# First expert tile from the first eleven token tiles, records loaded one tile deeper, another stage order in the head

## The reference

```python
# token phase, both parts
scores = scale * np.matmul(q_c, k_c.transpose(0, 1, 2, 4, 3))      # chunks of 64 of 576, 8 x 8 heads, d = 64
attn = softmax(scores)                                              # written out in the reference, eps 1e-9
x = (attn @ v_c), laid out as 4608 tokens x 512
r = np.maximum(x @ w_in, 0.0)                                       # 512 -> 2048
x2 = (s * (r * r) + b) @ w_out                                      # 2048 -> 512
# expert phase
do_compute = x2 @ w_skip > 0
logits = x2[do_compute] @ w_gate                                    # 8 experts
e_idx, gate_w = argmax(logits), softmax(logits) at e_idx
for e in range(8):
    y = gate_w * (np.maximum(x2[of e] @ w1[e], 0.0) @ w2[e])        # 512 -> 1024 -> 512
    out[of e] = x2[of e] + y
out[not do_compute] = x2
```

## Time and profile before

| | us |
|---|---|
| median of 3 runs | 1430.13 |
| lowest, highest | 1428.49, 1430.82 |
| the profiled execution | 1431.54 |
| its span in the trace | 1429.8 |

### The profile page before, as it was taken

One profiled execution on the slowest core, in us unless ns is written; L12 is line 12 of the kernel. 1 busy time (PEld: TensorE's weight loads), 2 busy tenths in 40 slices (PEclk: granted clock), 3 DMA queues, 4 the chain that ended last, 5 costly groups with the idle time before them and its releaser, 6 DMA issues.

```text
span 1429.8 us, 22258 instructions
## 1 busy us (share of the span) xinstructions
PE 1338.8 (94%) x7002; PEld 1175.2 (82%) x7003; DVE 937.3 (66%) x2130; ACT 776.3 (54%) x1900; POOL 339.4 (24%) x284
## 2 busy tenths in 40 slices
PE   3699999999999999999999999998578899999998
PEld 3698999989898989889898989997466777888887
DVE  3586878878796878778786978756355655233332
ACT  5696766657575757666575756543344543222221
POOL 4552222122222222121222222101121222111111
PEclk9899999999999999999999999999799999999999
DMA  5142212112031203112121302023454641111110
GB/s 210 67 148 89 100 34 91 44 40 93 31 100 27 94 23 100 35 62 69 42 93 29 104 19 89 31 95 126 154 184 153 239 162 37 44 39 42 43 44 25
DMA packets 61459, 116.25 MB, mean 81 GB/s; under 512 B 11704, under 2 KB 20920, under 8 KB 61216
## 3 DMA queue, kind: packets, MB, share of 16 engines
q1 hardware_dynamic: 40816, 73.51, 15.8%
q10 hardware_dynamic: 14416, 27.79, 5.6%
q0 software_dynamic: 6112, 13.56, 2.9%
HBM read 90.49 MB, written 27.08 MB: 82 GB/s over the span
## 4 chain that ended last, share of the span: by engine, by line
PE 72%; issue 10%; DMA 6%; POOL 5%; DVE 4%; ACT 2%; DVEq 1%; POOLq 0%; ACTq 0%; SPq 0%
PE h_ps L645 22%; PE y_ps L660 22%; PE y_ps L763 10%; PE h_ps L750 8%; PE s_ps L608 3%; DMA wide<-x_rows,got 3%; PE av_ps L626 3%; POOL qk_lo L491 2%; DMA got<-table 2%; POOL table L510 2%; PE t_ps L743 1%; PE t_ps L616 1%; ACT soft L834 1%; PE av_ps L757 1%; DVE weights_lo L1024 1%
## 5 line engine op out<-in xcount | busy, mean ns | idle before, releaser
L1051 DVE CUSTOM_DVE_ANT_0 products<-scratch,wide 128x512 f32<-128x512 f32 x297 | 302.3, 1018 | 6.6
L645 PE MATMUL h_ps<-rows_t_hi,weights_lo 128*128 128x384 f32 x768 | 261.5, 340 | 7.3 <-issue 5.5
L864 ACT ACTIVATE scratch<-h_ps 128x384 f32<-128x384 f32 x192 | 94.5, 492 | 307.2 <-PE h_ps L645 305.2
L645 PE MATMUL h_ps<-rows_t_hi,weights_hi 128*128 128x384 f32 x768 | 260.6, 339 | 0.0
L645 PE MATMUL h_ps<-rows_t_lo,weights_hi 128*128 128x384 f32 x768 | 259.2, 337 | 0.0
L660 PE MATMUL y_ps<-weights_hi,g_lo 128*128 128x512 f32 x576 | 227.1, 394 | 0.6 <-DVE g_lo L1030 0.6
L660 PE MATMUL y_ps<-weights_hi,g_hi 128*128 128x512 f32 x576 | 226.7, 394 | 0.0
L660 PE MATMUL y_ps<-weights_lo,g_hi 128*128 128x512 f32 x576 | 226.5, 393 | 0.0
L1030 DVE TENSOR_TENSOR g_lo<-scratch,g_hi 128x384 fp32r<-128x384 f32 x192 | 109.3, 570 | 104.0 <-ACT g_hi L812 101.7
L491 POOL TENSOR_TENSOR qk_lo<-qk_raw,qk_hi 128x768 fp32r<-128x768 f32 x66 | 128.4, 1945 | 146.0 <-ACT qk_hi L812 146.0
L645 PEld LDWEIGHTS h_ps<-rows_t_hi,weights_lo 128*128 128x128 f32 x768 | 145.2, 189 | 21.1 <-issue 7.1
(11 more groups left out here) (168 smaller groups left out, 2445.4 us busy)
## 6 DMA issues: line engine op xcount, KB each, us to landing
qk_raw<-in_qk SPq DMA_DIRECT2D x66, 384.0 KB, 3.0
expert_raw<-in_w ACTq DMA_DIRECT2D x32, 512.0 KB, 5.0
scratch<-in_w ACTq DMA_DIRECT2D x21, 512.0 KB, 5.3
out<-scratch SPq DMA_DIRECT2D x12, 768.0 KB, 4.2
x_rows<-scratch SPq DMA_DIRECT2D x12, 768.0 KB, 6.0
v_raw<-in_v SPq DMA_DIRECT2D x66, 128.0 KB, 2.1
expert_raw<-in_w SPq DMA_DIRECT2D x11, 512.0 KB, 3.8
wide<-in_w_out SPq DMA_DIRECT2D x7, 512.0 KB, 4.1
```

The lines of the kernel that those rows point to most:

```text
L645: mm = pe.matmul(h_ps[f % 2][:, 0:TOK], w[:, f // PAIR, kt, fs], x[:, z, kt, :], start=kt == 0 and n == 0, stop=kt == KT - 1 and n == 2)
L864: act.activation(r_buf[f % 2], h_ps[f % 2][:, 0:TOK], ACT.Relu).then_inc(r_done, 1)
L1051: dve.tensor_tensor_reduce(products[:, :], x2_sb[:, t, :], gate_w[:, e, :], 1.0, 0.0, ALU.mult, ALU.add, logits[:, t, e:e + 1]).then_inc(d ...
```

## The change

1. **Head.** The orders of the stages per step are B, D, C instead of D, B, C on the matmul engine, A, D, C, B instead of D, A, C, B on ScalarE, and B, D, C, B2 instead of D, B, C, B2 on VectorE.
2. **Token tiles.** ScalarE takes stage A ahead of the parts of g in slot 1. The last value product stands after 3 instead of 6 matmuls of its slot's `into_h`. In the last token tile routing of tile 10 is finished in slot 9 instead of 14, with three dots a slot.
3. **First expert tile.** Expert tile 0 takes the first 128 records of expert 0 as they stand after eleven token tiles. `next_row` of expert 0 is raised to at least 128, so that later tokens go to the next expert tile; expert 0 gets at least two tiles. Its records are loaded and its rows gathered within the last token tile, and it is computed between the logits and the bounds of that tile, written out as straight code. The loops over experts begin at expert tile 1.
4. **Records.** A new copy `idx` of the records serves the gather, so that `got` is free as soon as `idx` is taken, and SP loads records one tile ahead. VectorE makes the copy (`next_records`), at the end of `stage_rows`, after a wait on its own two copies and on the record load.
5. **Weights.** Expert 1's first three pieces are loaded at the start of the last token tile, the fourth ahead of the last store, pieces 4 to 6 after it; the staging places of expert 0 move accordingly. The order of the last loads on SP is new; ScalarE's queue no longer issues four of them between the phases.

The diff, cut to its core:

```diff
@@ tensor
-                for stage, c in first_chunks(step, ("D", "B", "C")):
+                for stage, c in first_chunks(step, ("B", "D", "C")):
@@ scalar
-                for stage, c in first_chunks(step, ("D", "A", "C", "B")):
+                for stage, c in first_chunks(step, ("A", "D", "C", "B")):
-                    order = "DCgAB" if f == FT - 1 else "CgADB"
+                    order = {1: "AgCDB", FT - 1: "DgCAB"}.get(f, "CgADB")
@@ vector
-                for stage, c in first_chunks(step, ("D", "B", "C", "B2")):
+                for stage, c in first_chunks(step, ("B", "D", "C", "B2")):
@@ tensor, slot 14
-                        into_h(i, f + 1, z, range(KT // 2))
+                        into_h(i, f + 1, z, range(1))
                         attention("D", CPT * (i + 1) + CPT - 1, CPT - 1)
-                        into_h(i, f + 1, z, range(KT // 2, KT))
+                        into_h(i, f + 1, z, range(1, KT))
@@ routing's slots
-        RANK_AT = 14
+        RANK_AT = {True: 14, False: 9}
...
+                by.append(min(by[-1] + (3 if f % 2 or not attend else 1), DOTS))
@@ sync
             sp.wait_ge(av_done, CPT * TILES)
-            for j in range(EXPERT_JOBS):
-                if j >= 2:
-                    sp.wait_ge(raw2_done, j - 1)
-                load_weights(sp, 0, j)
-            store_rows(TILES - 1)
-            sp.wait_ge(raw2_done, EXPERT_JOBS)
+            sp.wait_ge(x_ready, CPT * TILES)
+            load_weights(sp, 0, 0)
+            load_weights(sp, 0, 1)
             for j in range(3):
                 load_weights(sp, 1, j)
-
-            def load_records(tile, row):
-
-                sp.wait_ge(got_free, tile + 1)
-                sp.dma_start(got[:, :], table[bass.ds(row, P), :]).then_inc(got_in, 16)
-
+            for j in range(2, EXPERT_JOBS - 1):
+                sp.wait_ge(raw2_done, j - 1)
+                load_weights(sp, 0, j)
+            sp.wait_ge(records_out, 16 * SUB * (TILES - 1))
+            load_records(0, 0)
+            sp.wait_ge(raw2_done, EXPERT_JOBS - 2)
+            load_weights(sp, 0, EXPERT_JOBS - 1)
+            sp.wait_ge(raw2_done, EXPERT_JOBS - 1)
+            load_weights(sp, 1, 3)
+            store_rows(TILES - 1)
+            sp.wait_ge(x2_stored, 32 * TILES)
+            sp.wait_ge(tail_done, 1)
+            for j in range(4, EXPERT_JOBS - 1):
+                load_weights(sp, 1, j)
+            sp.wait_ge(bounds_ready, 1)
+            first_end = sp.value_load(bounds[0:1, 1:2], min_val=2, max_val=N // P + E)
             sp.wait_ge(records_out, 16 * SUB * TILES)
-            sp.wait_ge(bounds_ready, 1)
-            with sp.Fori(0, E) as e:
+            with sp.Fori(1, first_end) as t:
+                load_records(t, t * P)
+            with sp.Fori(1, E) as e:
...
@@ gpsimd
-            send_records(TILES - 2)
-            send_records(TILES - 1)
-            pool.memset(x_rows, 0.0).then_inc(rows_held, 16)
+            def gather(count, stored):
+                pool.wait_ge(x2_stored, 32 * stored)
                 pool.wait_ge(rows_held, count)
                 pool.indirect_dma_start(
-                    in_offset=bass.IndirectOffsetOnAxis(ap=got[:, 0:1].bitcast(U32), axis=0),
+                    in_offset=bass.IndirectOffsetOnAxis(ap=idx[:, 0:1].bitcast(U32), axis=0),
...
-            pool.wait_ge(bounds_ready, 1)
-            gather(16)
-            pool.dma_start(y_rows, x2_rows[0:P, :]).then_inc(y_free, 16)
-            gather(32)
+            send_records(TILES - 2)
+            pool.wait_ge(dots_done, DOTS * (TILES - 1))
+            pool.memset(x_rows, 0.0).then_inc(x_blank, 1)
+            pool.wait_ge(x2_stored, 32)
+            pool.dma_start(y_rows, x2_rows[0:P, :]).then_inc(y_free, 16)
+            pool.wait_ge(x_blank, 1)
+            gather(16, TILES - 1)
+            send_records(TILES - 1)
+            gather(32, TILES)
+            pool.wait_ge(bounds_ready, 1)
@@ tensor: behind the token tiles
-            pe.wait_ge(bounds_ready, 1)
+            pe.wait_ge(route_step, ROUTE_STEPS * (TILES - 2) + RANKS_READ)
             turn_rows(0)
...
             pe.wait_ge(raw2_done, EXPERT_JOBS // 4)
             first_half(0, 1)
+            rank(TILES - 1)
+            turn_h(0, 0)
+            pe.wait_ge(raw2_done, EXPERT_JOBS // 2)
+            up(1, 1)
+            pe.wait_ge(raw2_done, EXPERT_JOBS)
+            pe.wait_ge(hl_done, 1)
+            down(1, range(0, 2))
+            turn_h(0, 1)
+            down(1, range(2, ET // 2))
+            pe.wait_ge(hl_done, 2)
+            down(1, range(ET // 2, ET))
+            pe.wait_ge(bounds_ready, 1)
+            turn_rows(1)
+            first_half(1, 1)
@@ vector: last token tile
+                    if not attend and f == RANK_AT[attend]:
+                        dve.wait_ge(route_step, ROUTE_STEPS * i)
+                        dve.tensor_scalar(next_row[:, 0:1], next_row[:, 0:1], float(P), None, ALU.max).then_inc(first_closed, 1)
+                        dve.wait_ge(first_closed, 1)
+                    if not attend and f == FT - 2:
+                        dve.wait_ge(got_in, 16)
+                        dve.tensor_copy(idx[:, :], got[:, :]).then_inc(rows_held, 16)
@@ vector: expert tiles
+            def next_records(k):
+                dve.wait_ge(got_in, 16 * k + 16)
+                dve.tensor_copy(idx[:, :], got[:, :]).then_inc(rows_held, 16)
             def stage_rows(k):
                 dve.wait_ge(rows_in, 16 * k + 16)
                 if not isinstance(k, int):
                     dve.wait_ge(rows_taken, k)
-                dve.tensor_copy(x_next, x_rows).then_inc(rows_held, 16)
-                dve.tensor_copy(next_held[:, :], got[:, :]).then_inc(got_free, 1)
+                dve.tensor_copy(x_next, x_rows)
+                dve.tensor_copy(next_held[:, :], idx[:, :]).then_inc(next_ready, 1)
+                dve.wait_ge(next_ready, k)
+                next_records(k + 1)
@@ vector: behind the token tiles
             lo_of_x(0)
-            stage_rows(0)
-            dve.wait_ge(got_free, 2)
-            dve.tensor_copy(sent[:, :], next_held[:, :]).then_inc(y_ready, 32)
-            take_rows(0)
+            split2(0, 1, EXPERT_JOBS - 1)
+            dve.wait_ge(rows_in, 16)
+            dve.tensor_copy(x_held, x_rows)
+            dve.tensor_copy(held[:, :], idx[:, :]).then_inc(rows_taken, 1)
+            dve.wait_ge(rows_taken, 1)
+            dve.tensor_copy(sent[:, :], held[:, :]).then_inc(y_ready, 32)
...
+            lo_of_h(0, 0)
...
+            lo_of_h(0, 1)
+            next_records(1)
+            finish(0)
+            lo_of_x(1)
+            stage_rows(1)
+            take_rows(1)
```

161 lines of the change are left out of this document (84 added, 77 removed).

## The result

The changed kernel took **1385.29 us** (median of 4 runs, 1384.13 to 1386.57), the kernel before 1430.47 beside it: a ratio of 0.9686, 95% interval 0.967 to 0.9703. Forecast were 1385, range 1376 to 1406.

What follows compares the result with a forecast made beforehand. The matmul engine is busy almost throughout, so only its waits can yield time: 5 + 3.8 + 13.6 - 1 + 23.6 = 45.0 us off a span of 1429.8 gives 1384.8, median near 1385; range 1376 to 1406.

Steps and rivals of the forecast that it cites:

- A: Rival, expert tiles: gather instructions stay shut out beside VectorE's splits, deeper records worth nothing, 1409 us; chance 0.19.
- B: Rival: gathers take 2 to 3 us longer or the gap saves 7, not 13; 1398 us; chance 0.17 with D.
- C: Rival, expert tiles: the record copy holds VectorE up while waiting for its load, 1435 us at the least; chance 0.02.
- D: Rival, last token tile: tile 0 starts late behind SP's queue; price 0 to 13 us, chance 0.17 together with B.
- Head, 5: Head: scores ahead of the value product shorten chunk periods from 6.94, bounded by ScalarE; 5 us, bounds 2 and 6.
- Token tiles, 3.8: Token tiles: copying low parts ahead of g's activations in slot 1 removes 0.39 us waits; 3.8 us, bounds 0 and 3.9.
- Slot 14: Token tiles: last value product brought forward by three matmuls finds its inputs ready over 2 us early; gain 0.
- Gap, 12.6: Between token and expert phases: tile 0 computed inside the routing chain saves 13.6 us, less 1 for new straight-line code.
- Records, 23.6: Expert tiles: records loaded a tile deeper nearly remove waits for gathered rows; 23.6 us, bounds 16 and 26.
- part 3: The gap between phases: tile 0 computed early, inside the routing chain, leaving a 5.6 us wait for tile 1's rows; 13.6 us.
- pair 2.35, then 0.9: Expert tiles: the gather instruction waits out the first pair of splits, 2.35 us, and ends 0.9 later.
- the allowance of 1.6: Expert tiles: 1.6 us taken off 25.2 for gathers that still come a little late.

Runs made afterwards that it cites:

- experiment 7: Changed kernel with VectorE's copy of the next records, which releases the gather, moved behind the second pair of splits: 1398.46 us, ratio 0.9786.
- experiment 1: Kernel before with only the head's three stage orders changed: 1428.28 us, ratio 0.9969.
- experiment 5: Changed kernel with four of expert 1's eight weight pieces split ahead of expert tile 1, expert 0 outside the loop: 1381.81 us, ratio 0.9674.
- experiment 4: Kernel before with only the records loaded one tile deeper, through the extra copy for the gather: 1407.08 us, ratio 0.9828.
- experiment 3: Kernel before with only slot 14 changed, the last value product behind one of four k steps of into_h instead of two: 1430.22 us, ratio 0.9992.
- experiment 9: Kernel before with head order, slot 1, slot 14, ScalarE's last-slot order and deeper records, without the early first tile: 1393.55 us, ratio 0.9746.
- experiment 11: Repeat on another chip of the changed kernel with four of expert 1's pieces split ahead of tile 1: 1382.75 us, ratio 0.967.
- experiment 6: Changed kernel with tile 1's records asked for ahead of expert 1's weight pieces 4 to 6: 1385.42 us, ratio 0.9695.

## Why the prediction was right, step by step

**What bounds it, and where the time comes from**: right. The places are those named, each with its sign, and the entry in the waits that was to come, VectorE's subtraction, came, as one grown from 2.2 to 5.7 and not as a new one. None of the rivals came about: no gather was shut out (A) or late (B), the record copy never waited over 0.2 in the expert tiles (C), and tile 0 started straight behind the last token matmul (D). A's condition, made true in experiment 7, gave 1398.46.

**Head, 5**: 5.1 in the trace, 4.4 in the time. The total is right, its steps are not. Each "of four full periods" was to shrink from 6.94 to 5.4, bounded by ScalarE. There were three such periods, two of which fell to 4.5, under that bound, and one rose to 7.46 behind GpSimd's split of weights (experiment 1). That the sum came out was luck.

**Token tiles, 3.8**: the failed step. The stop was priced by its idle time, 0.39, and called the whole of it; start to start it was 0.57, and 0.67 with the next matmul, in 11 tiles instead of 10. By the period, 0.65 a tile, that is 7.2. Slot 14, forecast at 0, can't be told from 0. The remaining 1.7 lies at the loop's crossings, in the main the third, where the kernel before had the lower clock and the changed kernel had not; no term of the forecast stood for it, and it is no work of the token tiles' new order. The prediction had noted for expert tiles that "a stop costs more than its idle time", and did not apply it here.

**Gap, 12.6**: 12.1 in the trace. Right were the 8.18 from transposed rows to the transpose of h (8.16 measured), and the wait behind tile 0 (5.6 forecast, 6.10 measured). Wrong were two terms that the kernel before could not show: the ranks behind `first_half`, 1.31 at the lower clock and 0 at the higher, and the table's write, 5.29 for 3.77, whose cause stays open. Against them stood the logits, read 5.4 after the last token matmul where 6.3 were forecast, and SP's loads of bounds, which gave 1.8 for 1.0.

**Records, 23.6**: the mechanism and its size were right (23.7 alone), the step that failed is "expert sizes make tiles 4, 5 and 6 splitting ones in a row". They do, but tile 0's early end makes tiles 1 and 2 another such pair. The order of splits was taken from the old trace, although part 3 of the same prediction had taken tile 0 out of the loop. Tile 2 is 1.8 of the 2.8 that came short; experiment 5 moved half of the splits and got 0.5 of that back. For the 1.0 outside tile 2 no cause is shown. Inside the term, the gather's wait was overestimated: "pair 2.35, then 0.9" was to end it after the pair, and it ended before the pair did. No gather came late, so the allowance of 1.6 stood for the right sum by a wrong reason (experiment 4).

Too little by 5.2 in the head and the token tiles and 0.5 at the end, too much by 2.7 in the records and 0.5 in the gap: 2.5 in all between the traces, and 0.3 between the medians, since the profiled execution of before was 1.1 above its median and that of the changed kernel 1.2 below. Errors of 5.7 one way and 3.2 the other left 2.5, and the two profiled executions happened to lie 2.3 further apart than the medians: the places and their signs were foreseen, the exact hit was luck.

**The skill's rule.** The Trainium skill (SBUF — State Buffer, "SBUF: two separate sides") has the ports that GpSimd and VectorE share as an exclusive lock, held for a whole instruction by whoever starts first. For a VectorE operation with two SBUF inputs, as a split is, it says so only against a GpSimd instruction that reads SBUF, and its warning about descriptors is written for another kind of VectorE operation; the prediction left both conditions out. The gather's instruction has its indices in SBUF, and the trace agrees with a lock on it: in experiment 7 and the earlier trace rows it ended 0.9 after a run of splits. Who gets the ports at the end of one split with the next one ready, that section does not say. In the changed kernel GpSimd got in at the first end, in experiment 7 it lost three.

## What to carry to other kernels

Price a stop of a busy engine by starts, from the instruction ahead of it to the one behind, and check it on the period of the loop: with modelled ends the idle time read 0.39 where 0.67 was lost. When a piece of work is taken out of a loop, ask which of its companions stay in it, since they now fall into the next pass and may meet work that used to have that pass to itself. And where GpSimd writes descriptors beside VectorE, ask for them where few operations with two SBUF inputs follow: ahead of a pair it cost nothing here, ahead of a run of four it cost 14 us over one phase. Last, look at the granted clock of both kernels stretch by stretch before a difference is put down to an edit: 1.7 us of this one stood in a stretch that no edit was aimed at.

## What the runs showed of the hardware

A gather's instruction that began within a split ended 0.88 to 0.92 after the end of a split, in every case (undisturbed it takes 1.02). Which split's end, the traces don't explain. In the changed kernel and in experiment 4 it was each time the split that it had begun in, 0.88 to 0.96 after that split's start, and the next one ran on. In experiment 7 (five times) and in the earlier trace rows it was the last of a run of four, and the instruction took 5.16 to 5.51. Neither the moment nor the length of the run decides. GpSimd's and VectorE's timeline of experiment 3:

```profile
1184.82 2.09 POOL L570 DMA_INDIRECT wide<-x_rows,got  x1 [6.58 <-DMA got<-table]
...
1184.79 2.35 DVE L1024 TENSOR_TENSOR weights_lo<-scratch,weights_hi 128x1024 fp32r<-128x1024 f32 x2
1187.06 2.35 DVE L1024 TENSOR_TENSOR weights_lo<-expert_raw,weights_hi 128x1024 fp32r<-128x1024 f32 x2
```

It began 0.02 into the first of four, as the one of the earlier trace rows did (0.03), and ended 0.9 after the first. Likewise one that began 0.37 into such a run took 1.75 (1108.55 in experiment 1), where experiment 7 has 5.17 for 0.36. The splits themselves kept their pace each time (1.14 from one to the next).

The granted clock fell to the lower level behind a stop of 1.82 to 2.02 us at the third crossing of the loop in four kernels, and not behind one of 1.87 in experiment 9. In the stretch from 980 to 985 us it was 0.66 in one execution of a kernel (experiment 11) and 1.00 in another of the same (experiment 5).

A write of 128 small records took 3.5 to 3.9 us to land in one family of kernels and 3.6 to 5.4 in the other, with the DMA system all but idle beside it in the changed kernel and in experiment 6.
